# Moving the query scores of an attention and feed-forward kernel from the seventh pair's products to the fourth pair's

## The chip, the cores and the metric

The kernel runs on one core of one Trainium2 chip, in one launch. The metric is the device time of that core in microseconds: the median of three runs of the kernel before, 944.77 us.

## The reference

Two batches of 12480 tokens of 128 channels; 49 agents per batch; then a feed-forward layer of 2048 features over all 24960 tokens.

```python
def _attn_ref(q, k, v, agents):
    scale = 1.0 / np.sqrt(q.shape[-1])
    def sm(a, b):
        s = scale * (a @ b.transpose(0, 2, 1))
        s = s - s.max(-1, keepdims=True)
        e = np.exp(s)
        return e / (e.sum(-1, keepdims=True) + 1e-09)
    a2k = sm(agents, k)
    agent_v = a2k @ v
    q2a = sm(q, agents)
    return q2a @ agent_v

def _moe_ref(x, w_in, w_out, alpha):
    h = x @ w_in
    g = np.maximum(h, 0.0) + alpha * np.minimum(h, 0.0)
    return g @ w_out
```

The output is `_moe_ref` of the attention's result, reshaped to tokens by channels.

## The kernel before, in words

**The algebra.** The attention of the queries to 49 agents is linear in `agent_v`, so the product `agent_v @ w_in` is made once per batch (`M_a`, `M_r`: the "mix") and each chunk of queries needs only its 49 weights per token. The activation is split into a linear part (`L_a`, `L_b`) and a part behind a ReLU. Numbers that must be more exact than fp16 are held as a high and a low part: `r_hi` is the fp16 of the hidden values, `r_lo` what is missing, and likewise `w_hi` and `w_lo`.

**The chunks.** There are 52 chunks `n` of 480 queries (4 tiles of 120). The function `body` treats two of them (`half` 0 and 1); `each_body` calls it 26 times on every engine. Each call has a kind: KEYS and TOP (chunks 0 to 11, which also compute the second batch's key scores), VALUES (12 to 19, the second batch's values), SUMS, MIX and MIX_REST (20 to 25, its mix), and PLAIN (26 to 51). Several bodies run in a hardware loop, those of the chunks 28 to 47 among them.

**One chunk on TensorE.** Hidden features come in 8 pairs of 128-row tiles. For each group of two pairs TensorE makes four tiles (`tiles`, line 539) and their remainder (`rest_of_quad`, line 546, which raises `h_ready`). ScalarE takes each pair out of PSUM as `r_hi` (`relu_hi`, line 875), and VectorE makes `r_lo` from PSUM and `r_hi` (`relu_lo`, line 1116, which raises `lo_ready`). Then TensorE makes six second-layer products for the pair (`second_layer`, line 556) into the bank OUT. PSUM has three slots of two banks for hidden pairs, so tiles of a pair wait for the low part of the pair that had their slot. The order on TensorE in a chunk is: tiles of the pairs 2 and 3 (pairs are counted from 0 in the code); products 0 and 1; tiles 4 and 5; products 2 and 3; the linear term (`linear`, line 566, in slot 0); tiles 6 and 7; products 4 and 5; tiles 0 and 1 of the next chunk; products 6 and 7. In words "the fourth pair" is pair 3 and "the seventh pair" is pair 6.

**The queries.** The scores of chunk `n + 3` are made in chunk `n`, four tiles of fp32 (`query_score`, line 520) into the bank SMALL, each tile behind one of the first four products of pair 6. SP loads the queries of chunk `n + 3` at line 297, at the top of its turn for chunk `n`, behind the store of the output of chunk `n - 1` (line 316), which waits for GpSimd's sum `y` (line 392); that waits for ScalarE's `y_relu` (line 954), which waits for the last product of chunk `n - 1`. VectorE's `query_shift` (lines 1093 and 1095) takes the maxima and subtracts them; it stands at the top of the next chunk. ScalarE's exponential follows behind the high part of pair 2, VectorE's sums and normalisation behind the low part of pair 2. The weights go through `stack`, are transposed by DMA into `PT` and copied into `PR` (lines 275 and 279, SP's `turn`).

**The bank SMALL.** It holds, in turn, the query scores and one other thing, by kind: key scores (line 708), value products (line 714 and 720), the key maxima, the sums, the pieces of the mix (line 501) and its remainder (line 508). TensorE waits for a semaphore of the reader (`k_saved`, `av_added`, `m_low`, `r_low` and others) before it writes the bank again. TensorE is in order: a wait stops everything behind it.

Of the kernel before, what the change touches and what calls it, by code (L numbers as in the profile page):

```python
# [19 lines left out]
FULL = N // (8 * KT)  # L20
# [17 lines left out]
EARLY = 2  # L38
# [3 lines left out]
def build(nc, kT, kTail, vP, vS, vTail, qT, agT, w_inT, w_out, alpha_col, out):  # L42
    ctx = ExitStack()
    with ctx:
# [359 lines left out]
        def _(pe):  # L404
# [252 lines left out]
            def body(i, b, kind):  # L657
                for half in range(2):
# [41 lines left out]
                    if kind == MIX:  # L700
                        pe.wait_ge(b_av, 2)
                        mix(1, 2 * half, SMALL)
                    if kind == MIX_REST and half == 0:
                        mix_rest(1, SMALL)
# [35 lines left out]
                    second_layer(3, half)  # L740
# [8 lines left out]

                    if kind == TOP and half == 0:  # L750
                        pe.wait_ge(k_saved, 2 * FULL + 2)
                        key_max_rows(1, SMALL)
                    if kind == SUMS and half == 1:
                        pe.wait_ge(b_dened, 2)
                        value_sums(1, SMALL)
                    if kind == MIX:
                        pe.wait_ge(m_low, 5 + 2 * half)
                        mix(1, 2 * half + 1, SMALL)
                    if kind == MIX_REST and half == 0:
                        pe.wait_ge(r_low, 2)  # L760
# [18 lines left out]
                    if not there(n + 3):  # L779
                        second_layer(6, half)  # L780
                    else:
                        pe.wait_ge(in_q[1 - half], 16 * i + 32 + 16 * half)

                        if kind == KEYS:
                            pe.wait_ge(k_saved, n + (FULL + EARLY + 2))
                        if kind == TOP and half == 0:
                            pe.wait_ge(b_diag, 2)
                        if kind == TOP and half == 1:
                            pe.wait_ge(b_shift, 2)
                        if kind == VALUES:  # L790
                            pe.wait_ge(av_added, n + (1 - FIRST_VALUES))
                        if kind == SUMS and half == 0:
                            pe.wait_ge(av_added, SECONDS + 1)
                        if kind == SUMS and half == 1:
                            pe.wait_ge(b_vmax, 2)
                        if kind == MIX:
                            pe.wait_ge(m_low, 6 + 2 * half)
                        if kind == MIX_REST and half == 0:
                            pe.wait_ge(l_low, 2)

                        def scores(t):
# [497 lines left out]
```

## Time and profile before

| What | us |
|---|---|
| Median of three runs | 944.77 |
| Lowest and highest of the three | 943.59, 946.69 |
| The profiled execution's own time | 946.44 |
| Its span in the profile | 944.3 |
| Mean granted TensorE clock, share of full speed | 0.991 |

The profile is of one execution. Its span runs from the first to the last recorded instruction; its own time has 2.1 us more around it. PE is TensorE's matmuls, PEld its weight loads (recorded apart, and able to run beside a matmul), DVE VectorE, ACT ScalarE, POOL GpSimd, SP the queue that issues nearly all DMAs. Of a chain of waits, each step is the one that released the next.

### The profile page before, as it was taken

To read this page: it belongs to the slowest core of one execution; us is meant where nothing else is said; L and a number is where in the kernel's file an instruction comes from. 1 tells how busy PE (TensorE), PEld (TensorE's weight loads), DVE (VectorE), ACT (ScalarE), POOL (GpSimd) and SP (SyncE) were. 2 spreads that over 40 slices of the span, in tenths; PEclk is the share of its full clock that TensorE was granted. 3 is DMA by queue.
4 is the path that set the end of the run, shared out by engine and by line. 5 is a ranking of instruction groups with operands and counts; after the bars stand their busy time and mean duration, and the time that the engine had idled before them with its cause. 6 is when DMAs were issued, how large, how long until landed. Compare 5 with 4: busy or idle time off the path is not lost.

```text
span 944.3 us, 16025 instructions
## 1 busy us (share of the span) xinstructions
PE 923.7 (98%) x5642; PEld 489.3 (52%) x5642; DVE 635.8 (67%) x927; ACT 514.4 (54%) x694; POOL 108.6 (11%) x140
## 2 busy tenths in 40 slices
PE   7899999999999999999999999999999999999998
PEld 7775555555545655655444444444444444444443
DVE  4567666676777777776767666666666666666664
ACT  2235555655565555555565555555555555555554
POOL 5320010100101100101001010101010101010101
PEclk9799999999999999999999999999999999999999
DMA  8752231232222322211111111111111111111110
GB/s 288 279 160 69 60 99 57 65 90 59 71 86 70 95 91 70 88 33 40 51 38 56 34 50 42 49 43 47 43 40 52 39 53 39 51 39 52 40 33 22
DMA packets 63205, 65.75 MB, mean 70 GB/s; under 512 B 38528, under 2 KB 57280, under 8 KB 62912
## 3 DMA queue, kind: packets, MB, share of 16 engines
q1 hardware_dynamic: 62880, 65.19, 22.7%
q8 instruction: 24, 0.39, 0.2%
q14 instruction: 13, 0.11, 0.0%
q10 hardware_dynamic: 288, 0.06, 0.0%
HBM read 40.49 MB, written 12.78 MB: 56 GB/s over the span
## 4 chain that ended last, share of the span: by engine, by line
PE 82%; DVE 7%; issue 5%; ACT 4%; DMA 1%; DVEq 0%; SPq 0%; POOLq 0%; ACTq 0%
PE ps L556 45%; PE ps L539 17%; PE ps L546 7%; DVE r_lo L1116 5%; ACT r_hi L875 4%; PE ps L520 3%; PE ps L407 2%; PE ps L714 2%; PE ps L708 1%; PE ps L483 1%; DMA kv_s<-kT 1%; PE ps L566 1%; PE ps L431 1%; PE ps L501 1%; PE ps L438 0%
## 5 line engine op out<-in xcount | busy, mean ns | idle before, releaser
L1116 DVE SCALAR_TENSOR_TENSOR r_lo<-ps,r_hi 128x960 f16<-128x960 f32 x416 | 466.6, 1153 | 259.2 <-ACT r_hi L875 256.7
L875 ACT ACTIVATE r_hi<-ps 128x960 f16<-128x960 f32 x416 | 386.1, 967 | 186.8 <-PE ps L546 186.7
L556 PE MATMUL ps<-r_hi,w_hi 128*128 128x480 f16 x832 | 252.3, 369 | 0.8 <-DVE q_e L1095 0.8
L556 PE MATMUL ps<-r_hi,w_lo 128*128 128x480 f16 x832 | 248.2, 367 | 0.0
L556 PE MATMUL ps<-r_lo,w_hi 128*128 128x480 f16 x832 | 240.9, 366 | 0.0
L539 PE MATMUL ps<-PT,M_a 128*128 128x480 f16 x832 | 211.6, 367 | 2.9 <-DVE r_lo L1116 0.7
L392 POOL TENSOR_TENSOR y<-y_relu,y_lin 128x480 f32<-128x480 f32 x52 | 62.4, 1199 | 626.2 <-ACT y_relu L954 451.8
L539 PEld LDWEIGHTS ps<-PT,M_a 128*128 128x128 f16 x832 | 77.0, 98 | 101.6 <-DVE r_lo L1116 27.8
L556 PEld LDWEIGHTS ps<-r_hi,w_lo 128*128 128x128 f16 x832 | 91.2, 110 | 68.7
L556 PEld LDWEIGHTS ps<-r_lo,w_hi 128*128 128x128 f16 x832 | 85.4, 106 | 71.2
L556 PEld LDWEIGHTS ps<-r_hi,w_hi 128*128 128x128 f16 x832 | 76.9, 106 | 86.3 <-issue 46.0
L546 PE MATMUL ps<-PR,M_r 32*128 32x480 f16 x624 | 78.7, 372 | 0.0
L546 PE MATMUL ps<-PT,M_r 32*128 32x480 f16 x208 | 77.3, 372 | 0.0
L520 PEld LDWEIGHTS ps<-agents,q_s 128*120 128x120 f32 x416 | 70.8, 187 | 4.1 <-issue 0.4
L954 ACT ACTIVATE y_relu<-ps,out_unscale 128x480 f32<-128x480 f32 x52 | 34.3, 660 | 64.8 <-PE ps L556 64.8
L520 PE MATMUL ps<-agents,q_s 128*120 128x49 f32 x416 | 64.9, 242 | 0.0
L937 ACT ACTIVATE y_lin<-ps,lin_unscale 128x480 f32<-128x480 f32 x52 | 34.3, 660 | 55.0 <-PE ps L566 55.0
L546 PEld LDWEIGHTS ps<-PT,M_r 32*128 32x128 f16 x208 | 18.9, 91 | 82.7 <-issue 82.2
L867 ACT ACTIVATE stack<-q_p 120x196 f16<-120x196 f32 x52 | 19.4, 373 | 62.1 <-DVE q_p L1107 62.1
L373 POOL TENSOR_TENSOR stack<-stack,ones 120x120 f16<-120x120 f16 x52 | 20.8, 400 | 181.3 <-ACT stack L867 181.3
L714 PEld LDWEIGHTS ps<-S,kv_s 128*128 128x128 f32 x192 | 33.2, 190 | 1.3
L974 DVE TENSOR_REDUCE k_top<-S 128x49 f32<-128x392 f32 (+2 forms) x26 | 20.0, 774 | 17.7 <-ACT S L827 17.7
(143 smaller groups left out, 546.7 us busy)
## 6 DMA issues: line engine op xcount, KB each, us to landing
q_s<-qT SPq DMA_DIRECT2D x52, 240.0 KB, 2.6
out<-y SPq DMA_DIRECT2D x52, 240.0 KB, 2.0
kv_s<-kT SPq DMA_DIRECT2D x24, 512.0 KB, 4.3
kv_s<-vP SPq DMA_DIRECT2D x12, 512.0 KB, 7.0
kv_s<-vS SPq DMA_DIRECT2D x8, 768.0 KB, 4.3
PR<-PT SPq DMA_DIRECT2D x156, 32.0 KB, 1.9
PT<-stack SPq DMA_TRANSPOSE x208, 2.4
w_lin<-w_out SPq DMA_DIRECT2D x1, 1024.0 KB, 7.8
```

What stands on the lines that cost most here:

```text
L373: pool.tensor_tensor(stack[0:T, :, 2 * A:128], stack[0:T, :, REST:A], ones[0:T, 0:4 * SPARE].rearrange("p (t a) -> p t a", a=SPARE), ALU.m ...
L392: pool.tensor_tensor(y[:, half, :], y_relu[:, half, :], y_lin[:, half, :], ALU.add).then_inc(y_ready, 1)
L520: return pe.matmul(ps[0:T, SMALL, t * A:(t + 1) * A], q_s[:, half, t * T:(t + 1) * T], agents[:, b * A:(b + 1) * A], start=True, stop=True)
L539: pe.matmul(by_tile(ps[:, 2 * slot(p) + u, 0:CHUNK]), M_a[:, b, f:f + 128], tokens(PT, half), start=True, stop=False)
L546: mm = pe.matmul(by_tile(ps[:, 2 * slot(2 * q + u // 2) + u % 2, 0:CHUNK]), M_r[32 * u:32 * u + 32, b, q * 128:(q + 1) * 128], tokens(src[ ...
L556: mm = pe.matmul(ps[:, OUT, 0:CHUNK], w[:, 2 * p + u, :], r[:, s, u, :], start=(p == 0 and u == 0 and k == 0), stop=(p == PAIRS - 1 and u ...
L714: mm = pe.matmul(ps[:, SMALL, 0:A], second_s[:, at:at + C], S[:, 1, SECOND * n + (t + 2 - SECOND * FIRST_VALUES), :], start=(t == 0), stop ...
L875: act.activation(r_hi[:, p % RING, :, :], ps[:, at:at + 2, 0:CHUNK], ACT.Relu).then_inc(hi_ready, 1)
L937: act.activation(y_lin[:, half, :], ps[:, 2 * LIN_SLOT, 0:CHUNK], ACT.Copy, scale=lin_unscale[:, b, :]).then_inc(lin_saved, 1)
L954: act.activation(y_relu[:, half, :], ps[:, OUT, 0:CHUNK], ACT.Copy, scale=out_unscale[:, b, :]).then_inc(relu_saved, 1)
L974: dve.tensor_reduce(k_top[:, b, m, :], by_agent(piece(b, m)), AX.X, ALU.max).then_inc(k_maxed, 1)
L1116: dve.scalar_tensor_tensor(out=r_lo[:, p % RING, :, :], in0=ps[:, at:at + 2, 0:CHUNK], scalar=0.0, in1=r_hi[:, p % RING, :, :], op0=ALU.ma ...
```

## The change

The four score tiles of chunk `n + 3` move from the products of pair 6 to the products of pair 3, in the same chunk `n`, with the wait for the query load and the waits for the other users of the bank SMALL. `query_shift` of chunk `n + 3` moves on VectorE from the top of the next chunk to behind the low part of pair 5 of this one. Behind the products of pair 4, the steps of the kinds TOP, SUMS, MIX and MIX_REST that write SMALL wait for `q_shifted`, since the scores are now in the bank before them.

```diff
                     if kind == MIX:
                         pe.wait_ge(b_av, 2)
+                        if half == 1:
+                            pe.wait_ge(m_low, 6)
                         mix(1, 2 * half, SMALL)
                     if kind == MIX_REST and half == 0:
+                        pe.wait_ge(m_low, 8)
                         mix_rest(1, SMALL)
...
                     pe.wait_ge(lo_ready, g + 4)
-                    second_layer(3, half)
+                    if not there(n + 3):
+                        second_layer(3, half)
+                    else:
+                        pe.wait_ge(in_q[1 - half], 16 * i + 32 + 16 * half)
+                        if keys:
+                            pe.wait_ge(k_saved, n + (FULL + EARLY + 2))
+                        elif kind == TOP:
+                            pe.wait_ge(b_shift, 2)
+                        elif kind == VALUES:
+                            pe.wait_ge(av_added, n + (1 - FIRST_VALUES))
+                        elif kind == SUMS and half == 0:
+                            pe.wait_ge(av_added, SECONDS + 1)
+                        elif kind == SUMS:
+                            pe.wait_ge(b_dened, 2)
+                        elif kind == MIX:
+                            pe.wait_ge(m_low, 5 + 2 * half)
+                        elif kind == MIX_REST and half == 0:
+                            pe.wait_ge(r_low, 2)
+                        elif kind == MIX_REST:
+                            pe.wait_ge(l_low, 2)
+                        else:
+                            pe.wait_ge(q_shifted, n + 3)
+
+                        def scores(t):
+                            if t < 4:
+                                scored = query_score(t, 1 - half, nb3)
+                                if t == 3:
+                                    scored.then_inc(q_scored, 1)
+
+                        second_layer(3, half, scores)
...
                     second_layer(4, half)
+                    if kind == TOP and half == 0 or kind == SUMS and half == 1 or kind == MIX or kind == MIX_REST and half == 0:
+                        pe.wait_ge(q_shifted, n + 4)
                     if kind == TOP and half == 0:
-                        pe.wait_ge(k_saved, 2 * FULL + 2)
                         key_max_rows(1, SMALL)
                     if kind == SUMS and half == 1:
-                        pe.wait_ge(b_dened, 2)
                         value_sums(1, SMALL)
                     if kind == MIX:
-                        pe.wait_ge(m_low, 5 + 2 * half)
                         mix(1, 2 * half + 1, SMALL)
                     if kind == MIX_REST and half == 0:
-                        pe.wait_ge(r_low, 2)
                         mix_linear(1, SMALL)
...
                     pe.wait_ge(lo_ready, g + 7)
-                    if not there(n + 3):
-                        second_layer(6, half)
-                    else:
-                        pe.wait_ge(in_q[1 - half], 16 * i + 32 + 16 * half)
...
-                        second_layer(6, half, scores)
+                    second_layer(6, half)
...
                     g = 2 * PAIRS * i + PAIRS * half
-                    if there(n + 2) and not (isinstance(n, int) and n == 0):
-                        query_shift(n + 2)
                     if kind == VALUES:
...
                     relu_lo(g + 4, 4)
                     relu_lo(g + 5, 5)
+                    if there(n + 3):
+                        query_shift(n + 3)
                     if kind == KEYS or kind == TOP and half == 0:
```

The order of the instructions, in a plain chunk. First TensorE, from the products of pair 2 to the tiles of pair 6 and 7 behind the linear term, as it was (`r_hi` and `r_lo` with `w_hi` and `w_lo` are the second layer, `PT` with `M_a` the tiles):

```order
L556 MATMUL ps<-r_lo,w_hi 128x480 x2
L556 MATMUL ps<-r_hi,w_hi 128x480 [waits lo_ready]
L556 MATMUL ps<-r_hi,w_hi 128x480
L556 MATMUL ps<-r_hi,w_lo 128x480 x2
L556 MATMUL ps<-r_lo,w_hi 128x480 x2
L566 MATMUL ps<-PT,L_a 128x480
L566 MATMUL ps<-PT,L_b 128x480
L539 MATMUL ps<-PT,M_a 128x480 [waits lo_ready]
L539 MATMUL ps<-PT,M_a 128x480
L539 MATMUL ps<-PT,M_a 128x480 [waits lo_ready]
```

And the same place with the change:

```order
L556 MATMUL ps<-r_hi,w_hi 128x480 [waits q_shifted,in_q1,lo_ready]
L520 MATMUL ps<-agents,q_s 120x49
L556 MATMUL ps<-r_hi,w_hi 128x480
L520 MATMUL ps<-agents,q_s 120x49
L556 MATMUL ps<-r_hi,w_lo 128x480
L520 MATMUL ps<-agents,q_s 120x49
L556 MATMUL ps<-r_hi,w_lo 128x480
L520 MATMUL ps<-agents,q_s 120x49
L556 MATMUL ps<-r_lo,w_hi 128x480 x2
L566 MATMUL ps<-PT,L_a 128x480
L566 MATMUL ps<-PT,L_b 128x480
L539 MATMUL ps<-PT,M_a 128x480 [waits lo_ready]
```

The four scores (line 520) stand between the products of pair 3, ahead of the linear term, and the first of these products now also waits for the query load (`in_q1`) and for `q_shifted`.

Second VectorE, through the same chunk, as it was (`q_top` and `q_e` are `query_shift`; `q_sum` to `q_p` the normalisation of an earlier chunk's scores):

```order
L1093 TENSOR_REDUCE q_top<-ps 120x4 [waits q_scored]
L1095 TENSOR_TENSOR q_e<-ps,q_top 120x196 [waits q_maxed]
L1116 SCALAR_TENSOR_TENSOR r_lo<-ps,r_hi 128x960 [waits hi_ready]
L1099 TENSOR_REDUCE q_sum<-q_e 120x4 [waits q_exped]
L1101 TENSOR_SCALAR q_den<-q_sum 120x4 [waits q_summed]
L1103 RECIPROCAL q_rec<-q_den 120x4 [waits q_dened]
L1107 TENSOR_TENSOR q_p<-q_e,q_rec 120x196 [waits q_reced]
L1116 SCALAR_TENSOR_TENSOR r_lo<-ps,r_hi 128x960 [waits hi_ready]
L1111 TENSOR_TENSOR stack<-q_p,stack 120x4x49 [waits q_hi]
L1116 SCALAR_TENSOR_TENSOR r_lo<-ps,r_hi 128x960 [waits hi_ready] x6
```

And with the change, where these lines stand four numbers lower in the file:

```order
L1120 SCALAR_TENSOR_TENSOR r_lo<-ps,r_hi 128x960 [waits hi_ready]
L1103 TENSOR_REDUCE q_sum<-q_e 120x4 [waits q_exped]
L1105 TENSOR_SCALAR q_den<-q_sum 120x4 [waits q_summed]
L1107 RECIPROCAL q_rec<-q_den 120x4 [waits q_dened]
L1111 TENSOR_TENSOR q_p<-q_e,q_rec 120x196 [waits q_reced]
L1120 SCALAR_TENSOR_TENSOR r_lo<-ps,r_hi 128x960 [waits hi_ready]
L1115 TENSOR_TENSOR stack<-q_p,stack 120x4x49 [waits q_hi]
L1120 SCALAR_TENSOR_TENSOR r_lo<-ps,r_hi 128x960 [waits hi_ready] x2
L1097 TENSOR_REDUCE q_top<-ps 120x4 [waits q_scored]
L1099 TENSOR_TENSOR q_e<-ps,q_top 120x196 [waits q_maxed]
L1120 SCALAR_TENSOR_TENSOR r_lo<-ps,r_hi 128x960 [waits hi_ready] x5
```

The maximum and the subtraction stood ahead of the low part of pair 2; they now stand behind those of the pairs 4 and 5, ahead of pair 6's. SP's order, GpSimd's and ScalarE's are what they were.

## Rows read from the trace of the kernel before

**Rows 1.** The page: busy time of each engine, with its share and instructions.
```profile
PE 923.7 (98%) x5642; PEld 489.3 (52%) x5642; DVE 635.8 (67%) x927; ACT 514.4 (54%) x694; POOL 108.6 (11%) x140
```

**Rows 2.** The page: the chain that ended last, by engine.
```profile
PE 82%; DVE 7%; issue 5%; ACT 4%; DMA 1%; DVEq 0%; SPq 0%; POOLq 0%; ACTq 0%
```

**Rows 3.** Waits: engine line waited for: us in total, times, longest us.
```profile
PEld ps L539 <- DVE r_lo L1116: 27.8, 54, 0.9
...
PEld ps L556 <- DVE q_e L1095: 1.3, 6, 0.2
```

**Rows 4.** Windows, us: busy (instructions) by engine, PEclk, DMA, GB/s.
```profile
600.95:616.83 15.88, 15.81 (x92) 7.39 (x90) 10.77 (x16) 9.21 (x12) 1.59 (x2) 1.00 0.17 45
907.03:922.24 15.21, 15.21 (x84) 6.45 (x82) 8.89 (x9) 8.65 (x10) 1.20 (x1) 1.00 0.10 30
```

**Rows 5.** Timeline, TensorE, plain chunk: start, us, line, out<-in [idle before].
```profile
606.54 0.38 PE L556 MATMUL ps<-r_hi,w_hi 128*128 128x480 f16 x1
...
607.96 0.57 PE L556 MATMUL ps<-r_lo,w_hi 128*128 128x480 f16 x2
...
613.24 0.97 PE L539 MATMUL ps<-PT,M_a 128*128 128x480 f16 x4
...
614.46 0.58 PE L556 MATMUL ps<-r_hi,w_hi 128*128 128x480 f16 x2
...
615.68 0.57 PE L556 MATMUL ps<-r_hi,w_hi 128*128 128x480 f16 x2
...
616.90 0.37 PE L566 MATMUL ps<-PT,L_a 128*128 128x480 f16 x1
...
617.30 1.22 PE L539 MATMUL ps<-PT,M_a 128*128 128x480 f16 x4
```

**Rows 6.** Timeline, TensorE, line 539: first chunk, second, and a plain one.
```profile
92.25 0.58 PE L539 MATMUL ps<-PT,M_a 128*128 128x480 f16 x2 [0.49 <-DVE r_lo L1116]
...
108.73 1.14 PE L539 MATMUL ps<-PT,M_a 128*128 128x480 f16 x4
...
871.37 1.21 PE L539 MATMUL ps<-PT,M_a 128*128 128x480 f16 x4
```

**Rows 7.** Timeline, VectorE, the same plain chunk.
```profile
607.75 2.22 DVE L1116 SCALAR_TENSOR_TENSOR r_lo<-ps,r_hi 128x960 f16<-128x960 f32 x2 [1.44 <-ACT r_hi L875]
609.88 0.35 DVE L1093 TENSOR_REDUCE q_top<-ps 120x4 f32<-120x196 f32 x1
610.27 0.36 DVE L1095 TENSOR_TENSOR q_e<-ps,q_top 120x196 f32<-120x196 f32 x1
...
615.66 2.22 DVE L1116 SCALAR_TENSOR_TENSOR r_lo<-ps,r_hi 128x960 f16<-128x960 f32 x2
619.96 2.22 DVE L1116 SCALAR_TENSOR_TENSOR r_lo<-ps,r_hi 128x960 f16<-128x960 f32 x2 [2.08 <-ACT r_hi L875]
```

**Rows 8.** Timeline, ScalarE, the same plain chunk.
```profile
614.66 1.83 ACT L875 ACTIVATE r_hi<-ps 128x960 f16<-128x960 f32 x2
```

**Rows 9.** Timeline, SP and weight loads, then line 297's landings (537 to 886).
```profile
609.20 1.83 SPq L279 DMA_DIRECT2D PR<-PT  x3
...
612.65 0.35 SPq L297 DMA_DIRECT2D q_s<-qT  x1
...
628.90 0.35 SPq L297 DMA_DIRECT2D q_s<-qT  x1
...
631.36 0.30 PEld L556 LDWEIGHTS ps<-r_hi,w_hi 128*128 128x128 f16 x2
...
DMA to landing us min/median/max: 2.3/2.6/3.2
```

**Rows 10.** Timeline: value chunk on VectorE; mixing chunk on VectorE and TensorE.
```profile
335.15 2.22 DVE L1116 SCALAR_TENSOR_TENSOR r_lo<-ps,r_hi 128x960 f16<-128x960 f32 x2 [1.40 <-ACT r_hi L875]
...
467.28 0.76 DVE L1068 SCALAR_TENSOR_TENSOR M_a<-M_a,gate,ps 32x512 f16<-32x512 f16 x1
...
468.66 0.57 PE L556 MATMUL ps<-r_hi,w_hi 128*128 128x480 f16 x2
```

More of the change, by code:

```diff
@@ L778, in body @@
                     pe.wait_ge(lo_ready, g + 7)
-                    if not there(n + 3):
-                        second_layer(6, half)
-                    else:
-                        pe.wait_ge(in_q[1 - half], 16 * i + 32 + 16 * half)
[L784 to L801, printed above, removed]
-                            if t < 4:
-                                scored = query_score(t, 1 - half, nb3)
-                                if t == 3:
-                                    scored.then_inc(q_scored, 1)
-                        second_layer(6, half, scores)
+                    second_layer(6, half)
                     pe.wait_ge(lo_ready, g + 8)
```

## The prediction

> **What bounds the kernel.** I read the busy shares first, then the chain that ended last, then the waits, and then the timeline of one chunk, engine by engine. TensorE's matmuls are busy for 98% of the span [rows 1], and the chain gives TensorE 82%, VectorE 7% and ScalarE 4% [rows 2]. So TensorE's own work sets the pace, and somewhere in each chunk a piece of VectorE and ScalarE comes onto the path. The waits say where: 54 times a weight load of the first-layer tiles (line 539) waited for a low part `r_lo`, 27.8 us in all, about once for each of the 52 chunks [rows 3].
>
> The timeline shows which tiles. Two second-layer products take 614.46 to 616.90, that is 2.44 us, and nothing waits in them. The group of four first-layer tiles at 613.24 lasts 0.97 us from its first start to its last end; the same four tiles at 617.30 last 1.22 [rows 5]. These are the tiles of the seventh and eighth pairs, and the second two of them wait for the sixth pair's low part, whose PSUM slot they take. I follow it back: the third group of hidden tiles is done when its products start at 614.46 [rows 5]; ScalarE starts the two high parts at 614.66 [rows 8]; VectorE starts the two low parts at 615.66 and ends at 617.88 [rows 7]. TensorE wants the slot after 2.44 us of products, 0.4 of the linear term and 0.4 of the first two tiles, at 617.70. The chain takes 3.4 us and the cover is 3.24, and a weight load has to be made after the wait. What the group loses is 1.22 - 0.97 = 0.25 us, in a chunk that now takes 15.88 us [rows 4]. The granted clock is 1.00 there [rows 4], so no part of this is the clock's.
>
> **What the change moves.** It adds and removes no instruction on any engine, and SP's order is the same. The four score tiles of a chunk stand between the products of the seventh pair: the first four of these products with the scores take 606.54 to 607.96, 1.42 us, where four products alone take 4 x 0.203 = 0.81 (a sixth of 2.44 / 2 each) [rows 5]. The scores thus cost 0.61 us of TensorE a chunk, and the windows agree: a chunk near the end without scores takes 15.21 us, where its own stretch is smaller by 0.07 [rows 4]. Moved to the fourth pair's products, they cost the same 0.61, but now they lie inside the cover of the late slot. The cover grows from 3.24 to 3.85 us, against a chain of 3.4 that has no step in it that depends on the scores. So the stretch of 0.25 should vanish, and 0.61 is more than enough for every size of it.
>
> **The sum.** The stretch is not equal in all chunks. Reading the row of this group in every chunk that has scores to move (49 of the 52), I find 34 of the kind at 871.37, of 1.21 or 1.22 us, and 14 of the kind at 108.73, of 1.13 or 1.14 [rows 6]. That is 34 x 0.24 = 8.2 us and 14 x 0.17 = 2.4 us. The first chunk is worse: TensorE itself is idle for 0.49 us before the second two tiles [rows 6] beside the hidden part of the wait, and I let it win the whole 0.6 of the scores. The last three chunks have no scores to move and keep their 0.17. Six weight loads of the second layer waited 1.3 us in all for `q_e`, the last step of the maxima [rows 3]; most of that is hidden in front of their matmuls, and with the maxima earlier by half a chunk it goes: I count 0.2. Together 11.4 us.
>
> **VectorE's part at no cost.** The maximum and the subtraction take 609.88 to 610.63, 0.75 us [rows 7]. Their new place is behind the sixth pair's low part, where VectorE sits idle for 2.08 us until the next high part [rows 7]; the 0.75 fits. The fullest such gap that I found steady is that of the value chunks, where a subtraction of 588 columns stands in it already and 1.40 us are left [rows 10]. If this cover were gone, the seventh pair's low part would be late, which the next chunk's second pair of tiles wait for. Where they leave, before the third pair's low part, VectorE waits for ScalarE's high part with or without them, so nothing is won there.
>
> **The cover that is taken away.** Without the scores, the seventh pair's products shrink by 0.61, and behind them the tiles of the next chunk's fourth pair wait for its first pair's low part. That low part starts 1.21 us after the tiles' group is done (606.54 to 607.75) and takes half of 2.22, ready at 2.32 [rows 5, 7]. The tiles come after two bare products and half a group, 2.44 + 0.4 = 2.84. Nearly 0.5 us is left, the same distance at which the group at 613.24 runs unstretched [rows 5], so I take nothing for it; below it the bound is 0, above it 0.24 a chunk, as much as the seen stretch.
>
> **The waits that come earlier.** The scores share a PSUM bank with the key scores, the value products and the mixing steps, so each of those must now be read out by the fourth pair's products. The tightest that I found is in the mixing chunks: the low part of the mix ends at 467.28 + 0.76 = 468.04, and those products start at 468.66 [rows 10]. 0.6 us are left, and it is a matter of four chunks; nothing. On TensorE everything is queued behind these waits, since they stand before the products and not before the scores.
>
> The query load is different. It is issued behind the store of the last chunk's output, and had 9.8 us until the seventh pair's products of its chunk (from 612.65 to 622.42, one period of 15.88 after 606.54); now the fourth pair's products need it. In an odd chunk it is issued at 612.65 and these products start at 615.68, 3.03 us later [rows 5, 9]. In an even chunk of the loop the issue comes later, at 628.90, while the first weight load of the products starts at 631.36 [rows 9]; the matmul behind it, one period of 15.88 after 615.68, is at 631.56, so the load has about 2.55 us. Loads of these chunks land 2.3 to 3.2 us after issue, 2.6 at the median [rows 9]. In the ten even chunks that pass the loop's end I take a wait of 0.05 us each, from the median, and for a single slow landing of 3.2 another 0.3: 0.8 us. The bounds are 0 (all at 2.3 to 2.5) and, if all 22 of the plain loop's chunks landed at 3.2, 11 x 0.65 + 11 x 0.25 = 10 us.
>
> The Trainium skill, page "DMA: Bandwidth & Descriptors", section "Anatomy of one DMA", gives about 2.0 us fixed plus the bytes at 436 GB/s; as an estimate from that page a 240 KB load takes 2.56 us. By that figure the even chunks would wait not at all or by a hair; the trace's median of 2.6 agrees [rows 9]. Its section "Rules for kernel authors" asks to issue a load early and wait for it late, which speaks against this change, since the lead shrinks; that rule becomes my second rival.
>
> The net gain is 11.4 - 0.8 = 10.6 us. The profiled execution took 946.44 us (a span of 944.3 and 2.1 around it), so it would become 935.8. The median of the three runs, 944.77, lies 1.7 below the profiled one, and against it the forecast is **934.2 us**.
>
> **The rivals.**
> - *The scores don't cover the wait.* The last chunks' own stretch speaks for it, since it is there with no scores and no work of the query on VectorE: perhaps a part of 0.17 belongs to the linear term's switch and not to a wait. Against it: weight loads are recorded as waiting for `r_lo`, 0.5 us each [rows 3], and the other groups run at 0.97. Then only 34 x 0.07 = 2.4 us go, less 0.8: 943. Chance 0.03.
> - *The query load is late, and the gain is partly or wholly eaten.* The load is issued right behind the store of 240 KB and shares the queue with it. If every plain chunk saw the slowest landing of 3.2, the 10 us worked out above would go, and the time is 944.8 - 11.4 + 10 = 943.4. For it: the 3.2 is in the rows; against it: so is the median of 2.6, with the same store in flight [rows 9]. Chance 0.06. The Trainium skill's rule (issue early, wait late) would have it this way.
> - *Slower than before.* The same wait, but with a landing that moves. The chunk is now shorter by 0.25, and SP has to finish the transposes and copies of the next query weights before it stores and loads. Should that delay the issue by a further 0.5 us or more in each chunk, a landing of 2.6 would cost 0.5 + 0.05 or more; over 24 plain chunks it breaks even with the 11.4 us at 0.48 a chunk, and at 0.8 a chunk gives 944.8 - 11.4 + 19 = 952. SP's copies are issued by 609.20 + 1.83 = 611.03, and the load at 612.65 with the store in between [rows 9]; that is room of a microsecond at most, of which the shorter cover takes 0.6, which is why this has a chance at all: 0.03.
> - *The stretch comes back at the taken cover*, at 0.24 a chunk: 944.8 - 11.4 + 0.8 + 49 x 0.24 = 946, no change. The 0.5 us of room speak against it: 0.04.
>
> **Numbers.** The forecast has 0.84. The range for 8 in 10 goes from 931.8 (all gains, no load wait, and a run 1.8 below the median's place; the runs before spread from 943.59 to 946.69) to 938.5 (a load wait of 0.2 us in each plain chunk, or half of the gain at the 14 smaller ones, with a run on the high side). A measurement of this kernel can tell about 0.3%, 2.8 us, from no change. Faster by more: the forecast, the partly late load and a little of the first rival, 0.91. Within it: 0.05. Slower: 0.04.
>
> **What would show it.** In the profile after, the chunk in the plain stretch should be 15.63 to 15.7 us instead of 15.88. The tile group behind the linear term should last 0.97 and its weight loads should not wait for `r_lo`, except in the last three chunks. The fourth pair's products with scores should take 1.8 us, the seventh's 1.2. New waits should be few: weight loads of line 556's products waiting for the query load, under 0.1 us each and in even chunks. VectorE's idle time behind the sixth pair's low part falls from 2.08 to about 1.7 with the maxima in it (TensorE's group comes some 0.4 us later against that low part). The forecast is wrong if the tile group keeps 1.1 or more, if the fourth pair's products wait for a DMA by 0.3 us and more in most chunks, or if another group of tiles stretches beyond 0.97.

## The result, and the profile after

The changed kernel takes **934.47 us** (median of 4 runs, 933.84 to 934.94), the kernel before in the same comparison 945.73 (4 runs, 943.59 to 946.84): a ratio of 0.9883, 95% interval 0.9862 to 0.9904. The profiled execution took 934.78 us, with a span of 933.1.

The page of the changed kernel: busy time by engine, and the chain by engine.

```profile
PE 913.1 (98%) x5642; PEld 489.6 (52%) x5642; DVE 636.1 (68%) x927; ACT 514.6 (55%) x694; POOL 108.7 (12%) x140
...
PE 92%; DVE 2%; DMA 2%; issue 2%; SPq 1%; ACT 1%; POOLq 0%; POOL 0%
```

TensorE's chain grew from 82% to 92%, and VectorE's fell from 7% to 2% [rows 1, 2]. TensorE's busy time fell by 10.6 us with the same 5642 matmuls: here a stretched group, as at 617.30 [rows 5], counts as busy for all of its time.

The waits (us in total, times, longest):

```profile
PEld ps L556 <- DVE r_lo L1120: 8.1, 37, 0.4
...
PEld ps L539 <- DVE r_lo L1120: 2.6, 5, 0.7
...
PE ps L556 <- DMA q_s<-qT: 1.1, 2, 0.7
```

The first-layer tiles' weight loads waited 54 times and 27.8 us for `r_lo` [rows 3]; now it is 5 times and 2.6 us. The query load is a new reason for TensorE to wait, twice. Weight loads of line 556 now wait for `r_lo` 37 times, 8.1 us: the products and not the tiles now come just as a low part ends. That is 0.2 us each, the same idle time that the loads have at other pairs of products, where the profile names no wait, and the matmuls are not late by it: the pair at 599.89 below is one of these, and it starts and lasts like the others.

Windows of one chunk each, from one linear term to the next (columns as in rows 4): a plain one and a key chunk of the changed kernel, and then a key and a value chunk of the kernel before.

```profile
578.91:594.61 15.70, 15.70 (x92) 7.38 (x90) 10.83 (x16) 9.21 (x12) 1.60 (x2) 1.00 0.16 46
123.42:140.30 16.88, 16.88 (x107) 9.44 (x106) 11.59 (x17) 9.66 (x13) 1.60 (x2) 1.00 0.24 75
```

```profile
125.00:142.12 17.12, 17.05 (x108) 9.37 (x107) 11.50 (x17) 9.65 (x13) 1.60 (x2) 1.00 0.25 74
349.82:367.67 17.85, 17.79 (x116) 10.36 (x115) 12.82 (x19) 9.85 (x13) 1.61 (x2) 1.00 0.28 87
```

A plain chunk that took 15.88 [rows 4] now takes 15.70 here, where the load makes it wait a little, and 15.63 or 15.64 in 17 of 23; a key chunk 16.88 instead of 17.04 to 17.12; a value chunk 17.50 (17.55 once) instead of 17.66 to 17.90.

TensorE's timeline of the next plain chunk, then VectorE's at its start:

```profile
595.01 0.97 PE L539 MATMUL ps<-PT,M_a 128*128 128x480 f16 x4
...
599.89 0.58 PE L556 MATMUL ps<-r_hi,w_hi 128*128 128x480 f16 x2
...
602.34 0.97 PE L539 MATMUL ps<-PT,M_a 128*128 128x480 f16 x4
...
608.44 0.37 PE L556 MATMUL ps<-r_hi,w_hi 128*128 128x480 f16 x1
...
610.25 0.37 PE L566 MATMUL ps<-PT,L_a 128*128 128x480 f16 x1
```

```profile
594.85 0.35 DVE L1097 TENSOR_REDUCE q_top<-ps 120x4 f32<-120x196 f32 x1
595.24 0.36 DVE L1099 TENSOR_TENSOR q_e<-ps,q_top 120x196 f32<-120x196 f32 x1
597.43 2.22 DVE L1120 SCALAR_TENSOR_TENSOR r_lo<-ps,r_hi 128x960 f16<-128x960 f32 x2 [1.83 <-ACT r_hi L879]
```

The group behind the linear term, 1.22 before [rows 5], lasts 0.97 (595.01), like the others. The products with the scores take 608.44 to 610.25, 1.81 us, and the bare pair 599.89 to 602.34, 2.45. The maximum and the subtraction stand at 594.85 and 595.24 behind the sixth pair's low part, and 1.83 us of idle time are left behind them, of 2.08 before [rows 7].

From the first second-layer product to the end of the span the kernel before took 944.3 - 81.57 = 862.7 us and the changed one 933.1 - 79.79 = 853.3: 9.4 us less. The other 1.8 us of the spans' difference lie ahead of that product, where the change has moved nothing; they are taken up at the end ("A clock dip ahead of the first product"). In what follows this stretch is called **the body**.

### The profile page after: what moved, and what is told of

It reads as the page before. It is cut to its first block, busy times and chain, and to the rows that moved or that the text cites. A ratio compares the mean times of both kernels' runs of the same rounds, so it can differ in the third digit from the quotient of the medians.

```text
span 933.1 us, 16065 instructions
## 1 busy us (share of the span) xinstructions
PE 913.1 (98%) x5642; PEld 489.6 (52%) x5642; DVE 636.1 (68%) x927; ACT 514.6 (55%) x694; POOL 108.7 (12%) x140
## 4 chain that ended last, share of the span: by engine, by line
PE 92%; DVE 2%; DMA 2%; issue 2%; SPq 1%; ACT 1%; POOLq 0%; POOL 0%
PE ps L556 54%; PE ps L539 17%; PE ps L546 7%; PE ps L520 3%; PE ps L566 2%; PE ps L718 2%; PE ps L407 2%; PE ps L712 1%; PE ps L483 1%; DMA kv_s<-kT 1%; PE ps L431 1%; PE ps L501 1%; DMA q_s<-qT 1%; SPq L275 0%; PE ps L438 0%
## 5 line engine op out<-in xcount | busy, mean ns | idle before, releaser
L539 PE MATMUL ps<-PT,M_a 128*128 128x480 f16 x832 | 203.3, 366 | 0.3 <-DVE r_lo L1120 0.2
L539 PEld LDWEIGHTS ps<-PT,M_a 128*128 128x128 f16 x832 | 81.1, 99 | 86.6 <-DVE r_lo L1120 2.6
L556 PEld LDWEIGHTS ps<-r_hi,w_hi 128*128 128x128 f16 x832 | 73.0, 106 | 85.3 <-issue 44.6
L712 PEld LDWEIGHTS ps<-agents,kv_s 128*128 128x128 f32 x176 | 30.9, 191 | 1.1
```

The source lines that it names most:

```text
L539: pe.matmul(by_tile(ps[:, 2 * slot(p) + u, 0:CHUNK]), M_a[:, b, f:f + 128], tokens(PT, half), start=True, stop=False)
L556: mm = pe.matmul(ps[:, OUT, 0:CHUNK], w[:, 2 * p + u, :], r[:, s, u, :], start=(p == 0 and u == 0 and k == 0), stop=(p == PAIRS - 1 and u ...
L712: mm = pe.matmul(ps[:, SMALL, t * A:(t + 1) * A], kv_s[:, half, t * KT:(t + 1) * KT], agents[:, A:2 * A], start=True, stop=True)
```

## The experiments

All times are medians; where a kernel's body is given, it is the span of its profile less the start of its first second-layer product. The kernel before measured 945.98 beside the first four runs, 945.88 beside the next four, and 945.33 beside the last two.

**The changed kernel again.**

> The changed kernel once more, timed in more rounds against the kernel before. In the two profiles the span fell by 11.2 us, but 1.8 us of it lie ahead of the first chunk's products, where nothing was changed. Theory of the cover (the scores fill the wait for the sixth pair's low part): what is real is 9.4 us in the bodies, so the ratio is about 0.990. If instead the change also made the part before the loops faster, the ratio is 0.988 or less and the part before the first products is again near 79.8 us.

Measured: 934.97 us (934.53 to 936.03), ratio 0.989 (0.9875 to 0.9906); body 853.1. Two waits for `q_s` come at the places at which the first profile has them, with 0.41 and 0.60 us of idle TensorE (0.42 and 0.71 there). They belong to the program. The ratio lies between the two that were expected, and the part ahead of the first product is again short (79.76); the last section takes it up.

**The query load a chunk earlier.** Where do these waits come from? SP's timeline of the changed kernel in the two chunks behind the mixing stage, the two products that waited, and the load's row in the list of DMAs (KB, median us to landing):

```profile
516.65 6.02 SPq L275 DMA_TRANSPOSE PT<-stack  x4
523.86 1.79 SPq L279 DMA_DIRECT2D PR<-PT  x3
525.70 0.58 SPq L316 DMA_DIRECT2D out<-y  x1
526.66 0.36 SPq L297 DMA_DIRECT2D q_s<-qT  x1
...
541.29 1.37 SPq L316 DMA_DIRECT2D out<-y  x1
542.90 0.36 SPq L297 DMA_DIRECT2D q_s<-qT  x1
```

```profile
529.29 0.37 PE L556 MATMUL ps<-r_hi,w_hi 128*128 128x480 f16 x1 [0.42 <-DMA q_s<-qT]
...
545.82 0.37 PE L556 MATMUL ps<-r_hi,w_hi 128*128 128x480 f16 x1 [0.71 <-DMA q_s<-qT]
```

```profile
q_s<-qT SPq DMA_DIRECT2D x52, 240.0 KB, 2.7
```

The load is issued at 526.66, behind four transposes of 6.02 us, the copies, and a store; the product that needs it should have started 0.42 before 529.29, which is 2.2 us behind the issue. One chunk on, the issue of the store takes 1.37 us (0.58 in the row above it), and the load goes out at 542.90, 2.2 before the time at which its product at 545.82 wanted it. The two landed 2.5 and 2.8 us after issue, beside the median of 2.7. It is the issue that is late; an odd plain chunk further on has 3.04 us between the two, an even one 2.66. In the kernel before the load of the first of these two chunks (SP) went out 3.14 us ahead of the same products (TensorE), that of the second 3.04 (549.13 and 552.17):

```profile
533.15 0.35 SPq L297 DMA_DIRECT2D q_s<-qT  x1
```

```profile
536.29 0.57 PE L556 MATMUL ps<-r_hi,w_hi 128*128 128x480 f16 x2
```

So the late issue came with the change: the four transposes ahead of the first took 5.46 us there and 6.02 here, the store's issue 0.36 and 0.37 there and 0.58 and 1.37 here. Why they take longer is not shown.

```diff
-                    if there(n + 3):
-                        sp.wait_ge(q_scored, n + 2)
-                        sp.dma_start(q_s[:, 1 - half, :], qT[n + 3]).then_inc(in_q[1 - half], 16)
+                    if there(n + 4):
+                        sp.wait_ge(q_scored, n + 3)
+                        sp.dma_start(q_s[:, half, :], qT[n + 4]).then_inc(in_q[half], 16)
```

The first such load, `qT[3]`, goes out ahead of the loop.

> The changed kernel, but SP loads the queries one chunk earlier (chunk n + 4 at the top of chunk n, into the buffer that chunk n + 2 has left). Theory of the late load: the waits of the fourth pair's products for the query load (0.59 and 0.88 us in the chunks 26 and 27, 0.03 to 0.10 in four others, 1.75 us in all) vanish, the time falls by 1.5 to 2 us against the changed kernel of this call, and every plain chunk takes 15.64 us. Rival: those two chunks were late for another cause (instructions fetched where the bodies change), and then 1.5 us of waiting stay in them under another name and the time is the same as the changed kernel's within 0.5 us.

Measured: **933.04 us** (932.42 to 933.84), ratio 0.9869 (0.9854 to 0.9885), 1.9 us under the changed kernel beside it; body 851.5. No wait for `q_s` is left after the start. Both chunks behind the mixing stage take 15.64, so the load was their whole delay, and the rival of the expectation is out. SP issues a load at the same place as before, but it is the next chunk's, and the product runs through at 528.12:

```profile
526.23 0.36 SPq L299 DMA_DIRECT2D q_s<-qT  x1
```

```profile
528.12 0.37 PE L558 MATMUL ps<-r_hi,w_hi 128*128 128x480 f16 x1
```

A second time, to see whether it holds:

> The changed kernel with the query load a chunk earlier, a second time. If the load's wait is the only thing it takes away, the median is again 933.0 within 0.6, about 1.5 to 2 us below the changed kernel's 934.5 to 935.0, with no wait for q_s in the loop. If the first result was a lucky set of runs, it comes out at 934.5 to 935.

Measured: 933.07 us (932.45 to 934.53), ratio 0.9875 (0.9859 to 0.9892), all plain chunks 15.63 or 15.64. It holds, and it is the fastest version here.

**The scores moved, the maxima left.** The new place of the scores alone: the maximum and the subtraction go back to the top of the next chunk, except in five special chunks in which the order forbids it.

```diff
+                    if there(n + 2) and not (isinstance(n, int) and n == 0) and not (
+                            kind == TOP and half == 1 or kind == MIX or kind == MIX_REST):
+                        query_shift(n + 2)
...
-                    if there(n + 3):
+                    if there(n + 3) and (kind == TOP and half == 0 or kind == SUMS and half == 1 or kind == MIX
+                                         or kind == MIX_REST and half == 0):
                         query_shift(n + 3)
```

> The changed kernel with the scores behind the fourth pair's products, but the maxima back at the top of the next chunk, except in the five chunks of the kinds TOP, SUMS, MIX and MIX_REST where a step behind them needs them early. Theory of the cover: where the maxima stand is worth 0 to 0.3 us (the few short waits for them in value chunks come back), so the time is the changed kernel's, and the tile group behind the linear term lasts 0.97 us. Rival, that the earlier maxima make the gain: the time goes back by 5 us or more, to 940 to 945.

Measured: 944.83 us (943.71 to 947.39, 11 runs), ratio 0.9994 (0.9983 to 1.0004); body 863.6. **This expectation fell to its rival, and with it a step of the prediction.** The stretch behind the linear term is gone (0.97 in the plain chunks, of 15.64 where the load makes none wait), and still the whole gain is lost: from the first linear term to the end of the mixing stage this kernel takes 435.4 us, the changed one 425.4. Key chunks take 17.3 to 17.4 instead of 16.88, value chunks 17.9 to 18.2 instead of 17.50. The waits (one of them, 0.8 us, stands ahead of the first product in every kernel here), then the place in one value chunk, on TensorE and VectorE:

```profile
PE ps L556 <- DVE q_e L1099: 6.3, 13, 0.8
PEld ps L556 <- DVE q_e L1099: 4.2, 6, 0.7
```

```profile
361.16 0.97 PE L539 MATMUL ps<-PT,M_a 128*128 128x480 f16 x4
...
363.03 0.37 PE L556 MATMUL ps<-r_hi,w_hi 128*128 128x480 f16 x1 [0.58 <-DVE q_e L1099]
```

```profile
362.06 0.35 DVE L1097 TENSOR_REDUCE q_top<-ps 120x4 f32<-120x196 f32 x1
362.44 0.36 DVE L1099 TENSOR_TENSOR q_e<-ps,q_top 120x196 f32<-120x196 f32 x1
```

And the same place in the kernel before:

```profile
358.38 0.97 PE L539 MATMUL ps<-PT,M_a 128*128 128x480 f16 x4
...
359.66 0.37 PE L556 MATMUL ps<-r_hi,w_hi 128*128 128x480 f16 x1
```

```profile
359.07 0.36 DVE L1095 TENSOR_TENSOR q_e<-ps,q_top 120x196 f32<-120x196 f32 x1
```

The first pair's products of a value chunk have value products between them (line 718, which is 714 in the kernel before), which write the bank from which VectorE reads the scores; so TensorE waits there for `q_e`. In the kernel before, `q_e` is done 1.05 us after the start of the tile group ahead of these products (359.07 + 0.36 - 358.38), and they start behind that group as good as at once. Here it is done 1.64 after it (362.44 + 0.36 - 361.16), since the seventh pair's products lost the scores' 0.61 us while VectorE's order is the old one, and the products start 0.58 late. The price of the scores' new place is thus a second late slot in every key and value chunk, and moving the maxima is what pays it.

**The maxima left in the plain chunks alone.** There nothing shares the bank at that place.

```diff
+                    if there(n + 2) and kind == PLAIN:
+                        query_shift(n + 2)
...
-                    if there(n + 3):
+                    if there(n + 3) and kind != PLAIN and not (kind == MIX_REST and half == 1):
                         query_shift(n + 3)
```

> The changed kernel with the maxima back at the top of the next chunk, but only for the scores made in the 22 plain chunks and the one before them. Theory from the run with the old maxima everywhere (the first pair's products of a chunk with keys or values write the scores' PSUM bank, so they wait for the maxima, and 0.61 us of cover has gone; a plain chunk writes nothing else there): nothing waits, the plain chunks take 15.64 us, the key chunks 16.88, and the time is the changed kernel's, within 0.5 us. Rival, that old maxima cost time wherever they stand: half of the loss comes back, 939 to 941 us.

Measured: 935.19 us (935.08 to 935.89), ratio 0.989 (0.9873 to 0.9908); body 853.3, as the changed kernel, with key chunks of 16.88 and value chunks of 17.50. So the maxima's place matters only where the bank is written at the first pair's products. Together with the run before: the moved scores give the group's stretch back, the moved maxima keep some 10 us from being lost again.

**One and two of the four score tiles moved,** with the maxima in their old place, and the five special chunks left as they were. One tile is 0.15 us of TensorE.

```diff
+                        def first(t):
+                            if t < 1:
+                                query_score(t, 1 - half, nb3)
+
+                        second_layer(3, half, first)
```

> As the run before it, but with one score tile moved and three left. Theory of the cover: 0.15 us of 0.24 is filled, so the group keeps a stretch of 0.09 us where it had 0.24 (it lasts 1.06 us), and none where it had 0.16; plain chunks take 15.73 us. The key chunks wait 0 to 0.1 us for the maxima, the value chunks 0.1 to 0.25: near 941 us. Rival, that the stretch is a matter of order and not of microseconds: it is 0 or 0.24, and the plain chunks take 15.64 or 15.88.

> The kernel before, with two of the four score tiles moved to the fourth pair's products and two left with the seventh's, maxima where they were (the five chunks of the kinds TOP, SUMS, MIX and MIX_REST in which another step writes the bank in between are left as they were). Theory of the cover: 0.30 us is more than the 0.25 that was missing, so the tile group behind the linear term is at 0.97 in every moved chunk, plain chunks take 15.64. The other cover loses 0.30 instead of 0.61, so key and value chunks wait 0.15 to 0.4 us for the maxima instead of 0.5 to 0.7: near 940 us. Rival, that the whole of the scores must stand in the cover: plain chunks at 15.76 or more.

Measured: one tile 941.35 us (940.09 to 942.24), ratio 0.9949 (0.993 to 0.9967), two tiles 941.55 (941.02 to 941.9), ratio 0.9955 (0.9941 to 0.9969). With one tile, the group behind the linear term keeps 0.09 of its 0.25 (first row, the kernel with one tile); with two it keeps nothing (second row, the kernel with two):

```profile
615.62 1.06 PE L539 MATMUL ps<-PT,M_a 128*128 128x480 f16 x4
```

```profile
616.71 0.97 PE L539 MATMUL ps<-PT,M_a 128*128 128x480 f16 x4
```

0.15 of added cover took away 0.16 of stretch, and where the stretch had been 0.17 it left 0.02 or less. With two tiles every moved chunk's group is at 0.97, and the plain chunks take 15.64, but for some that are longer by up to 0.17 and one of 16.39, where the load is waited for. That is the plainest proof of the chain against the cover: the stretch falls one for one until it is gone, and the rest of the four tiles buys nothing. That both come out only 4 us below the kernel before has mostly the reason found above, in part of its size: the key chunks stay at 16.9 to 17.1 and the value chunks at 17.5 to 17.9, together 4.0 us (two tiles) and 2.8 (one) more than in the changed kernel. The chunks 20 to 25, where most are unmoved, cost another 0.9 and 0.7.

**The scores one pair earlier still** (the third pair's products), to double the demand on the load.

```diff
-                        second_layer(2, half)
+                        second_layer(2, half, scores)
+                    pe.wait_ge(lo_ready, g + 4)
+                    second_layer(3, half)
```

> The changed kernel with the scores and their waits one place further up, behind the products of the third pair instead of the fourth. Theory of the cover: both places lie between the third group and the late slot, so the tile group behind the linear term stays at 0.97 us. Theory of the late load: the products that wait for it now start 1.22 us earlier, so a plain chunk waits about 1.3 us (even) and 0.8 us (odd) for it, near 25 us in all, and the time is about 959 us, slower than before by 1.5%. Rival, that loads are early enough and place does not matter: 934 to 936 us.

Measured: 967.12 us (964.8 to 968.44), ratio 1.0219 (1.0201 to 1.0236), slower than before by 2%. Waits, then SP and TensorE in one plain chunk:

```profile
PE ps L556 <- DMA q_s<-qT: 28.8, 29, 1.7
PEld ps L556 <- DMA q_s<-qT: 10.3, 11, 1.9
```

```profile
704.14 0.35 SPq L297 DMA_DIRECT2D q_s<-qT  x1
```

```profile
706.82 0.37 PE L556 MATMUL ps<-r_hi,w_hi 128*128 128x480 f16 x1 [1.17 <-DMA q_s<-qT]
```

The load goes out 2.68 us before its product starts, and of these 1.17 are idle. This is the rival "slower than before", one pair further on: it is real, and 1.2 us of lead separate the changed kernel from it. In the plain chunks the size came as expected too: they take 16.6 and 16.9 in turn, so each loses 0.9 to 1.3 us against 15.64, 23.9 in all against the changed kernel, where about 25 were expected. The 8 us by which the expectation was too low lie elsewhere: 1.6 in the first chunk, whose products wait 1.67 for the load, 2.3 in the other chunks with keys and values, and 4.2 in the six chunks up to the mixing stage's end, mostly for the shared bank.

The same order with the load a chunk earlier:

> The scores behind the third pair's products, as in the run that was slower than before, and the query load one chunk earlier. Theory of the late load: all waits for the load go (39 us in the profile of that run), what stays is the wait for the mix's low parts in four to five chunks, 0.5 to 0.7 us each, so the time is near 936 us and plain chunks take 15.64. Rival, that the third pair's place is bad in itself: it stays above 945 us.

Measured: 939.81 us (938.02 to 940.62), ratio 0.994 (0.9922 to 0.9957); body 856.4. All plain chunks are at 15.64, as with the fourth pair. So the load was the loss there, though the time is 4 us above the expected one. The body is 4.9 us longer than the best version's. 4.1 of it is the shared bank again: six chunks, the last key chunk, those before the mixing stage and the mixing chunks, are longer by 0.5 to 0.8 each. Another 1.0 is a load: that of the first chunk, issued just ahead of the loop, comes too late for the third pair. TensorE's timeline, three of the products that waited:

```profile
87.57 0.38 PE L558 MATMUL ps<-r_hi,w_hi 128*128 128x480 f16 x1 [1.11 <-DMA q_s<-qT]
...
430.13 0.36 PE L558 MATMUL ps<-r_hi,w_hi 128*128 128x480 f16 x1 [0.64 <-DVE av_acc L1228]
...
446.78 0.36 PE L558 MATMUL ps<-r_hi,w_hi 128*128 128x480 f16 x1 [0.71 <-DVE den L1040]
```

In the last two the readers of the bank (the attention sums, the denominators; in other chunks the shifted keys and the mix, 0.61 and 0.68) are not done by the third pair's products. It is the wait that I had looked for at the fourth pair and found 0.6 us away [rows 10].

**The kernel before, profiled again,** for the part ahead of the first product:

> The kernel before, profiled a second time, to see how far two profiles of one kernel differ. From the first second-layer product to the end of the span both theories expect what the first profile of it shows, 862.7 us within 0.2, and 15.88 us for a plain chunk, since that part repeats to 0.01 us per chunk. The part ahead of the first product is what is asked: if the 1.8 us by which the changed kernel was earlier there (79.8 against 81.6) is the clock's chance and no part of the change, this run may start its first product anywhere from 79.2 to 81.6, as the profiles of the other kernels did; if the change makes that part shorter, it starts near 81.6 again.

Measured: first product at 81.40, body 944.2 - 81.40 = 862.8, plain chunks 15.88. It is read in the last section.

## Why the prediction was right, and where it was not

The forecast was 934.2 and the result 934.47. The mechanism is the predicted one, but one step was missed, one term was mis-sized, and that the two numbers agree to 0.3 us is luck (the last point).

- *The stretch behind the linear term.* Right. The group went to 0.97 in 48 of the 49 chunks whose scores moved, and kept its old length in the last three, as the sum had it (1.14 at 906.99). In the first chunk it fell from 1.64 to 1.19 only, a gain of 0.45 where 0.6 was taken. The gain of 11.4 can be read by itself from the version without load waits: body 862.7 - 851.5 = 11.2 us. The `q_e` part of 0.2 is in it, in two value chunks that were 0.1 and 0.16 longer than the rest (one is the 17.85 above).

```profile
906.99 1.14 PE L539 MATMUL ps<-PT,M_a 128*128 128x480 f16 x4
```

- *The query load.* The term was 0.8 us and measured 1.75, by the length of the chunks above 15.64: the steady plain chunks gave 0.28 (four waits of 0.03 to 0.10), and the two right behind the mixing stage 0.59 and 0.88. The issue times were taken from the steady plain stretch, and there they held: 3.04 us of lead in odd chunks and 2.66 in even ones, where the prediction's 2.55 was a little short (631.56 - 628.90 = 2.66). Landings were as foreseen, 2.4 to 2.8. What failed is the assumption that the old lead holds in every chunk: the two loads behind the mixing stage had 3.14 and 3.04 us in the kernel before, no less than the steady ones, and 2.2 in the changed one. Rows of the kernel before could not have shown that; it is the delay of the issue that the third rival named, in two chunks and not in each. In the prediction's upper bound for this term, 0.25 in the odd chunks should be 3.2 - 3.03 = 0.17, and the bound 9 us and not 10; nothing else hangs on it. The estimate of 2.56 us from the Trainium skill, "DMA: Bandwidth & Descriptors", section "Anatomy of one DMA", is a fit to DMAs issued by GpSimd, and this load is issued by SP; it lies near the measured median all the same, and the sum did not use it.
- *"Nothing is won there"* (the maxima's old place) is the step that failed. For plain chunks it is true, as the run with the old place there shows. In the key and value chunks the early maxima are worth about 10 us, the whole of the gain. The forecast was not hurt, because the change moves both, and the term cancels: the cover taken from the first pair's products is given back by the earlier maxima. The prediction did not know that it needed them, so this too is luck.
- *The cover that is taken away.* I asked which tiles stand behind the shorter products, found 0.5 us there, and that was right: no group other than the one behind the linear term grew. I did not ask it of the bank that the same stretch protects.
- *The bank's earlier waits.* Right: nothing in the changed kernel, and six chunks longer by 0.5 to 0.8 us one pair earlier.
- *The rivals.* Scores that don't cover: ruled out by the one and two tiles. Load late in every chunk: not with this lead; with 1.2 us less of it, yes, and there it is slower than before. There the rule that the Trainium skill gives in "DMA: Bandwidth & Descriptors", section "Rules for kernel authors" (issue a load early and wait for it late) decides the sign. At the changed kernel's own place it is worth 1.9 us, measured with the early load. A stretch that comes back at the taken cover: it would have come in key and value chunks and at the products, not at the tiles.
- *The sum.* 10.6 us were predicted for the profiled pair. The body gave 9.4, 1.0 less by the load and 0.2 by the stretch; 1.8 came from ahead of the first product, which nothing in the prediction speaks of, and made the spans differ by 11.2. Besides, the forecast was set against a median of 944.77, and the kernel before measured 945.73 with its fourth run and 945.3 to 946.0 later. The errors offset each other: 945.73 - 10.6 + 1.2 - 1.8 is 934.5.

## What to carry to other kernels

When work is moved out of a stretch, list everything that the stretch gave time to: not only the next operation behind it, but each slot, bank and buffer that is handed over while it lasts, in each kind of iteration. A consumer may have to move along with its producer although it looks free where it is. And when a read moves earlier, don't carry its load's lead over from the old trace: read it again in the new one, in the iterations behind an unusual stage above all, since the issue can move too. A load that can be issued an iteration ahead costs nothing here and ends the question for all chunks of the changed kernel.

## What was not expected of the hardware

**A clock dip ahead of the first product.** The first products start at 81.57 and 81.40 us in the two profiles of the kernel before, and at 79.79 and 79.76 in two of the changed one, though the work up to there is the same. Windows (columns as in rows 4) and TensorE's timeline, for the kernel before, its second profile, the changed kernel, and the one with the scores at the third pair:

```profile
24.00:25.00 1.00, 1.00 (x6) 1.00 (x6) 0.00 (x0) 0.00 (x0) 0.00 (x0) 0.50 0.20 78
...
22.50 0.38 PE L455 MATMUL ps<-ident,w_col 128*1 128x128 f32 x2 [1.95 <-DVE w_col L1137]
22.80 3.29 PE L407 MATMUL ps<-agents,kv_s 128*128 128x128 f32 x16
```

```profile
24.00:25.00 1.00, 1.00 (x7) 1.00 (x5) 0.00 (x0) 0.00 (x0) 0.00 (x0) 0.50 0.02 8
...
22.60 2.74 PE L407 MATMUL ps<-agents,kv_s 128*128 128x128 f32 x16
```

```profile
24.00:25.00 1.00, 1.00 (x9) 0.87 (x8) 0.00 (x0) 0.19 (x1) 0.00 (x0) 1.00 0.12 41
...
22.41 0.38 PE L455 MATMUL ps<-ident,w_col 128*1 128x128 f32 x2 [1.95 <-DVE w_col L1141]
22.72 2.05 PE L407 MATMUL ps<-agents,kv_s 128*128 128x128 f32 x16
```

```profile
24.00:25.00 1.00, 1.00 (x7) 1.00 (x6) 0.00 (x0) 0.00 (x0) 0.00 (x0) 0.50 0.09 37
...
22.73 2.78 PE L407 MATMUL ps<-agents,kv_s 128*128 128x128 f32 x16
```

In all of them TensorE has been idle for 1.95 us, waiting for VectorE's `w_col`, when it starts at about 22.5. In the kernel before the granted clock is then at 0.50, the lower level of 1.2 GHz, from 23.4 to 26.8 (from 23.8 to 27.2 in its second profile), and the sixteen matmuls that take 2.05 us in the changed kernel take 3.29 and 2.74. In the changed kernel it stays at 1.00 there. Yet the kernel with the scores at the third pair, which has the changed kernel's instructions up to this point, has the lower clock as well, and starts its products at 81.51. So it is not what the change does that decides. Of the twelve profiles six have this stretch of lower clock, with the same idle time of 1.95 us ahead of it in all twelve.

Nor does it seem to belong to a kernel, though two profiles of each agree. Of 29 more executions of the kernel before, the 12 with a mean granted clock of 0.992 or more have spans of 941.7 to 943.6 us, and the 17 with 0.99 or 0.991 have 943.2 to 945.1; both its profiles are of the second kind. The kernel with the scores at the third pair and the early load has no such stretch in its profile (span 936.3, clock 0.993), and its three other executions have 938.1 to 938.9 at 0.991. These have no trace, so it is not shown that the stretch is what they differ by; but it looks as if an execution can have it or not, those of the kernel before more often (17 of 29 at the lower clock) than those of the changed kernel (3 of 8). The 1.8 us are no gain of the moved scores. At equal clock the spans differ by less than the medians do: 942.5 (median of nine) against 932.1 and 932.8 at 0.993, 944.1 (median of eleven) against 933.2 to 934.3 at 0.991, which is 9.7 to 10.9 us, where the bodies differ by 9.4 to 9.7. What decides the clock stays open.

**A late weight load hides some of its wait.** The loads of the stretched groups waited about 0.5 us each (27.8 us over 54), and the groups grew by 0.16 to 0.25 (0.67 in the first chunk, where TensorE itself stood idle for 0.49). Where the rest of the wait goes no run here shows.
